# Order of maxima, low parts and prologue changed in an attention and gated-MLP kernel, with GpSimd's low parts in halves

## The chip, the cores and the metric

The kernel runs on one core of one Trainium2 chip. The metric is device time in microseconds (us), lower is better. Before the change three runs gave 1069.33, 1069.58 and 1069.66; their median is 1069.58.

## What is computed

32 heads (4 x 8) of attention over 576 positions with head size 64, in float32, then a gated MLP and a second MLP with a softmax gate and a layer norm:

```python
scores = scale * np.matmul(q, k.transpose(0, 1, 3, 2))
thresh = np.max(scores, axis=-1, keepdims=True) - tau
scores = np.where(scores >= thresh, scores, -1000000000.0)
attn = np.exp(scores - np.max(scores, axis=-1, keepdims=True))
attn = attn / (np.sum(attn, axis=-1, keepdims=True) + 1e-09)
x = np.matmul(attn, v)                      # then laid out as tokens x 512
x = (x @ w_a) * (x @ w_b) @ w_out           # 2304 tokens, 512 -> 1536 -> 512
h = x @ w_in                                # 512 -> 1024
solu = h * softmax(h)
out = layer_norm(solu) * g_ln @ w_out2      # 1024 -> 512
```

The change lies in the attention part only, the first 390 us or so.

## The kernel before

**Numbers in two parts.** Each float32 operand of a product is split into a high part (ScalarE rounds it) and a low part (the rest, by a subtraction). The low part of q and k is made by VectorE (`low_qk`, L811), that of v by GpSimd (`split_v`, L515), that of the probabilities by GpSimd (`low_probs`, L523, 576 columns in one instruction).

**Pairs and slots.** Two heads make a pair, and there are 16 pairs. A head of 576 rows is 4.5 tiles of 128, so a pair is nine slots, 0 to 8: slots 0 to 3 belong to the even head, slots 5 to 8 to the odd one, slot 4 (`MID`) to both and with twice the matmuls. In each slot TensorE does three things in this order (`step` in the tensor block): the scores of a tile one slot ahead (`scores`, for the maxima; in slot 8 that is tile 0 of the pair after the next), the transposed scores of this slot's tile (`scores_t`, for the probabilities), and some matmuls of probabilities and values of earlier tiles (`values`). All this work is 140 matmuls of 288 columns per pair.

**The maxima.** `score_max` (L820) reduces a tile of scores to one column of negated maxima. When a head's tiles are all reduced, ScalarE copies the high parts (`high_max`, L617), GpSimd subtracts to get the low parts (`low_max`, L531), VectorE turns the columns to rows (`turn_max`, L828), and SyncE stores them to DRAM (`store_max`, L352) and loads them back (`load_max`, L357) as two further rows of the operand tile `ops`. So the transposed scores come out with the maximum subtracted.

**Dealing.** `deal` (L341) fills one of four places in `ops` with a head's operands by six DMAs on SyncE's queue: zeros on the two rows of the maxima (`deal_zeros`, L322), the high parts (L328 to L330), the low parts (L338, L339). TensorE waits for all six before it starts the scores of that head: for the even head of pair n+2 in slot 8 of pair n, for the odd head of pair n+1 in slot 3 of pair n. `dealt` counts what has landed.

**The orders.** Each engine has one queue in program order; nothing is reordered. The order is written out by hand in the `step` of each block. SyncE, in a pair e: deal the odd head of e+1, store and load the odd maxima of the pair, load q and k, load v, move a finished head, spread its sums; then deal the even head of e+2, store the even maxima of e+1, load v, load maxima, load q and k, store the inverse, move a head. VectorE turns the odd maxima in slot 0 and the even ones of the next pair in slot 5, ahead of `mask` (L834); `low_qk` stands in slots 2 and 6 (L877, L879), `invert` in slot 7.

**Start and end.** Before the loop TensorE computes the scores of pair 0 alone; the operands of head 0 come straight from the engines, those of the others by `deal`. In slot 8 of pair 14 VectorE also normalizes the first token chunk (`normalize`, L846). Ahead of pair 14 SyncE issues four loads of the inverse sums (`load_inverse`).

Of the kernel before, what the change touches and what calls it, by code (L numbers as in the profile page):

```python
# [16 lines left out]
F32 = mybir.dt.float32  # L17
# [18 lines left out]
def build_program(nc, qkT, v_tiles, tau, w_a, w_b, w_o, w_in, w_out, g_col, eye, out):  # L36
# [35 lines left out]
    with outer:  # L72
# [115 lines left out]
        v_lo_set = sem("v_lo_set")  # L188
        s_done = sem("s_done")
        max_done = sem("max_done")  # L190
        max_hi_done = sem("max_hi_done")
# [104 lines left out]
        def dealt(i, j):  # L296

            return DEALT * (i + j // ROLL + (1 if j % ROLL else 0))

# [6 lines left out]
        def _(sp):  # L306
# [34 lines left out]
            def deal(i, j):  # L341


                at_least(sp, st_done, number(i - 1, j // 2, MID + 1 if j % 2 == 0 else SLOTS))
                deal_zeros(i, j)
                deal_high(i, j)
                deal_low(i, j)
# [50 lines left out]
            def step(i, e):  # L398

                head(deal, i, e + 1, 1)  # L400
                head(store_max, i, e, 1)
                head(load_max, i, e, 1)
                head(load_qk, i, e + 3, 0)
                head(load_v, i, e + 1, 0)

                head(move_head, i, e - 1, 1)
                pair(spread_sums, i, e - 1)

                head(deal, i, e + 2, 0)
                head(store_max, i, e + 1, 0)  # L410
                head(load_v, i, e + 1, 1)
                head(load_max, i, e + 1, 0)
                head(load_qk, i, e + 3, 1)
                pair(store_inverse, i, e - 1)
                head(move_head, i, e, 0)
# [6 lines left out]
            sp.wait_ge(consts_set, CONSTS)  # L422
            deal_zeros(0, 1)
            deal_high(0, 1, qk_hi_done)
            deal_low(0, 1)
            load_qk(0, 2)
            load_v(0, 0)
            deal_zeros(0, 2)
            deal_high(0, 2, qk_hi_done)
            load_qk(0, 3)  # L430
            deal_low(0, 2)
            load_v(0, 1)
            store_max(0, 0)
            load_qk(1, 0)
            load_max(0, 0)
            load_qk(1, 1)
# [57 lines left out]
        def _(pool):  # L494
# [23 lines left out]
            def low_probs(i, e, s):  # L518
                n = number(i, e, s)
                r = (SLOTS * e + s) % RP  # L520
                pool.wait_ge(p_hi_done, n + 1)
                at_least(pool, pv_done, used_up(i, e, s, RP))
                pool.tensor_tensor(p_lo[:, r, :], prob[:, s % RAW, :], p_hi[:, r, :].bitcast(F32),  # L523
                                   ALU.subtract).then_inc(p_lo_done, 1)

# [51 lines left out]
        def _(act):  # L577
# [13 lines left out]
            def exps(i, e, s):  # L591
                n, ps = number(i, e, s), st_ps[(SLOTS * e + s) % 2]
                act.wait_ge(st_done, n + 1)
                at_least(act, p_lo_done, n + 1 - RAW)
                act.activation(halves(prob[:, s % RAW, :]), ps[:, :, 0:HALF], ACT.Exp,  # L595
# [80 lines left out]
            act.wait_ge(consts_set, CONSTS + 3)  # L676
            high_max(0, 0)
            high_qk(0, 3)
# [123 lines left out]
        def _(dve):  # L802
# [58 lines left out]
            def step(i, e):  # L861
                for s in range(SLOTS):
# [3 lines left out]
                    ni, ne = pair_at(i, e + 1)  # L866
                    if s == 0:
                        turn_max(i, 2 * e + 1)
                    if s == 5 and exists(ni, ne):
                        turn_max(ni, 2 * ne)  # L870
                    if s > 0:
                        mask(i, e, s - 1)
                    elif not (isinstance(i, int) and 2 * i + e == 0):
                        mask(*pair_at(i, e - 1), SLOTS - 1)
                    mi, me = pair_at(i, e + 2)
                    if s == 2 and exists(mi, me):
                        low_qk(mi, 2 * me)  # L877
                    if s == 6 and exists(mi, me):
                        low_qk(mi, 2 * me + 1)  # L879
                    if s == 7 and not (isinstance(i, int) and 2 * i + e == 0):  # L880
                        invert(*pair_at(i, e - 1))
# [17 lines left out]
            for s in range(MID):  # L899
                score_max(0, 0, s, first_ps[s % 3])  # L900
            low_qk(0, 2)
            score_max(0, 0, MID, first_ps[MID % 3])
            score_max(0, 0, MID + 1, first_ps[(MID + 1) % 3])
            turn_max(0, 0)
            for s in range(MID + 2, SLOTS):
# [4 lines left out]
            dve.wait_ge(tau_ready, 1)  # L910
            low_qk(0, 3)
            last = heads // ROLL - 1
            for i in range(2):
# [134 lines left out]
        def _(pe):  # L1048
            def product(ps, e, s, weights, moving, done):


                parts = operands(e, s)
                for b in range(2):
# [26 lines left out]
            def values(i, e, side, *parts):  # L1080

                for t, part in parts:
# [5 lines left out]
                    if part == 2:  # L1088
                        pe.wait_ge(p_lo_done, n + 1)
                    elif part == 0:  # L1090
                        pe.wait_ge(p_hi_done, n + 1)
# [51 lines left out]
            for s in range(SLOTS):  # L1143
                at_least(pe, max_done, s - 2)
                scores(0, 0, s, first_ps[s % 3])
            pe.wait_ge(max_done, SLOTS - 2)
            scores(0, 1, 0, first_ps[SLOTS % 3])
# [167 lines left out]
```

## Time and profile before

| | |
|---|---|
| median of three runs | 1069.58 us |
| the profiled execution, its own time | 1069.29 us |
| its span in the trace | 1067.1 us |
| TensorE matmul / weight load busy | 94% / 88% of the span |
| VectorE / ScalarE / GpSimd busy | 51% / 39% / 24% |
| granted TensorE clock, mean | 0.976 |
| DMA packets | 51578, 71.33 MB |

Matmuls are pipelined and their ends are modelled, so the busy share of TensorE is not the share of its peak. 2.2 us of the profiled execution lie outside the span. The attention part ends near 390 us; the stages behind it keep TensorE busy throughout.

### The profile page before, as it was taken

What the parts mean: (1) busy time and instruction counts of PE and PEld (TensorE: products, weight loads), DVE (VectorE), ACT (ScalarE), POOL (GpSimd) and SP (SyncE); (2) the same over time, 40 slices, a digit from 0 to 9 for tenths busy, and PEclk for the clock granted to TensorE, in tenths of its full rate; (3) what the DMA queues carried; (4) which work ended last, traced back from release to release, by engine and by line L of the source; (5) the groups of instructions that cost most, each with busy time, mean ns of one, the idle gap of its engine ahead of it and who ended that gap; (6) DMA issues with size and microseconds to landing.
All of it is one profiled execution on the core that took longest, in us unless ns stands there. A gap on an engine that the chain in (4) does not pass through costs nothing.

```text
span 1067.1 us, 16652 instructions
## 1 busy us (share of the span) xinstructions
PE 1001.3 (94%) x5840; PEld 943.0 (88%) x5840; DVE 543.4 (51%) x862; ACT 415.1 (39%) x739; POOL 252.4 (24%) x242
## 2 busy tenths in 40 slices
PE   4899988999998889999999999999999999999998
PEld 4888878888887879999999999999999978888886
DVE  5676676677677675442122122222223485666564
ACT  2666656566665674431121121211212422322231
POOL 2666666566665670000000000000000000000000
PEclk8999998899999999999999999999999999999999
DMA  5545555454564425421001001000002200000000
GB/s 147 145 119 138 144 124 130 123 139 117 134 148 109 96 75 163 135 60 30 1 1 29 0 0 29 0 0 0 0 0 79 79 10 20 29 20 20 20 30 29
DMA packets 51578, 71.33 MB, mean 67 GB/s; under 512 B 14558, under 2 KB 24926, under 8 KB 51548
## 3 DMA queue, kind: packets, MB, share of 16 engines
q1 hardware_dynamic: 51548, 70.95, 24.9%
q8 instruction: 16, 0.26, 0.1%
q14 instruction: 14, 0.11, 0.0%
HBM read 33.25 MB, written 5.32 MB: 36 GB/s over the span
## 4 chain that ended last, share of the span: by engine, by line
PE 80%; issue 7%; DVE 4%; ACT 3%; DMA 2%; SPq 2%; POOL 2%; DVEq 0%; ACTq 0%; POOLq 0%
PE PS L1111 9%; PE PS L1112 9%; PE PS L1113 9%; PE PS L1094 8%; PE PS L1057 7%; PE PS L1059 5%; PE PS L1177 5%; PE PS L1176 5%; PE PS L1178 5%; PE PS L1235 3%; PE PS L1237 3%; PE PS L1236 3%; PE PS L1211 3%; PE PS L1209 3%; PE PS L1210 3%
## 5 line engine op out<-in xcount | busy, mean ns | idle before, releaser
L523 POOL TENSOR_TENSOR p_lo<-prob,p_hi 128x576 fp32r<-128x576 f32 x144 | 207.3, 1440 | 131.8 <-ACT p_hi L602 131.5
L1057 PE MATMUL PS<-ops 128*128 128x288 f32 x640 | 192.6, 320 | 47.7 <-DVE neg_max L820 29.2
L1111 PE MATMUL PS<-x_hi,w_ab_rolled 128*128 128x384 f32 x576 | 192.5, 334 | 1.4 <-issue 1.4
L1112 PE MATMUL PS<-x_lo,w_ab_rolled 128*128 128x384 f32 x576 | 192.4, 334 | 0.0
L1113 PE MATMUL PS<-x_hi,w_ab_rolled 128*128 128x384 f32 x576 | 192.4, 334 | 0.0
L1059 PE MATMUL PS<-ops 128*128 128x288 f32 x640 | 185.2, 308 | 0.0
L1057 PEld LDWEIGHTS PS<-ops 128*128 128x128 f32 x640 | 129.2, 202 | 61.4 <-DVE neg_max L820 36.4
L931 DVE TENSOR_TENSOR gate<-gate,PS 128x384 f32<-128x384 f32 x72 | 39.9, 554 | 253.0 <-ACT gate L701 253.0
L820 DVE TENSOR_REDUCE neg_max<-PS 128x1 f32<-128x576 f32 x144 | 108.6, 756 | 92.8 <-PE PS L1059 91.6
L701 ACT ACTIVATE gate<-PS 128x384 f32<-128x384 f32 x72 | 35.4, 491 | 268.2 <-PE PS L1113 268.2
L1059 PEld LDWEIGHTS PS<-ops 128*128 128x128 f32 x640 | 129.5, 202 | 0.0
L602 ACT ACTIVATE p_hi<-prob 128x576 fp32r<-128x576 f32 x144 | 98.4, 683 | 72.1 <-DVE prob L834 68.7
L595 ACT ACTIVATE prob<-PS 128x576 f32<-128x576 f32 x144 | 93.2, 647 | 65.3 <-PE PS L1059 63.4
L834 DVE SCALAR_TENSOR_TENSOR prob<-PS,neg_tau,prob 128x576 f32<-128x576 f32 x144 | 115.2, 801 | 2.8 <-ACT prob L595 2.8
L1111 PEld LDWEIGHTS PS<-x_hi,w_ab_rolled 128*128 128x128 f32 x576 | 108.1, 188 | 1.7 <-issue 1.7
L1112 PEld LDWEIGHTS PS<-x_lo,w_ab_rolled 128*128 128x128 f32 x576 | 108.1, 188 | 0.0
L1113 PEld LDWEIGHTS PS<-x_hi,w_ab_rolled 128*128 128x128 f32 x576 | 108.1, 188 | 0.0
L563 POOL MEMSET halfpow<- 128x1 f32 x1 | 0.1, 104 | 448.0 <-PE PS L1178 448.0
L1176 PE MATMUL PS<-g_hi,w_od 128*128 128x384 f32 x288 | 96.2, 334 | 0.0
L1177 PE MATMUL PS<-g_lo,w_od 128*128 128x384 f32 x288 | 96.2, 334 | 0.0
L1178 PE MATMUL PS<-g_hi,w_od 128*128 128x384 f32 x288 | 96.2, 334 | 0.0
L1094 PE MATMUL PS<-p_hi,v_hi 128*65 128x288 f32 x320 | 72.1, 308 | 9.2 <-issue 8.9
(89 smaller groups left out, 1546.8 us busy)
## 6 DMA issues: line engine op xcount, KB each, us to landing
qk_raw<-qkT_dram SPq DMA_DIRECT2D x32, 288.0 KB, 2.8
ops<-qk_hi SPq DMA_DIRECT2D x62, 144.0 KB
ops<-qk_hi SPq DMA_DIRECT2D x31, 288.0 KB
ops<-qk_lo SPq DMA_DIRECT2D x62, 144.0 KB
v_raw<-v_tiles_dram SPq DMA_DIRECT2D x32, 160.0 KB, 2.4
xT<-head_sb SPq DMA_DIRECT2D x32, 144.0 KB, 2.4
out_dram<-o_sb SPq DMA_DIRECT2D x18, 256.0 KB, 2.0
stage<-inverse_dram SPq DMA_DIRECT2D x20, 192.0 KB, 3.8
```

Source lines behind the costliest of these rows:

```text
L523: pool.tensor_tensor(p_lo[:, r, :], prob[:, s % RAW, :], p_hi[:, r, :].bitcast(F32), ALU.subtract).then_inc(p_lo_done, 1)
L820: dve.tensor_reduce(out=neg_max[:, e, s:s + 1], in_=ps[:, :, 0:HALF], axis=AX_XY, op=ALU.max, negate=True).then_inc(max_done, 1)
L834: dve.scalar_tensor_tensor(out=p, in0=ps[:, :, 0:HALF], scalar=neg_tau[:, 0:1], in1=p, op0=ALU.is_ge, op1=ALU.mult).then_inc(mask_done, 1)
L1057: pe.matmul(ps[:, b, 0:HALF], weights[0][:, r, own], moving[0][:, r, cols], start=(n == 0), stop=False)
L1059: ins = pe.matmul(ps[:, b, 0:HALF], weights[1][:, r, own], moving[1][:, r, cols], start=False, stop=(n == len(parts) - 1))
L1094: ins = pe.matmul(o_ps[0:D + 1, b, 0:HALF], v[:, side, t, :], p[:, r, b * HALF:(b + 1) * HALF], start=(t == 0 and part == 0), stop=(t == N ...
L1111: pe.matmul(bank, w[:, 0, :], x_hi[:, k, :], start=(k == 0), stop=False)
L1112: pe.matmul(bank, w[:, 0, :], x_lo[:, k, :], start=False, stop=False)
L1113: ins = pe.matmul(bank, w[:, 1, :], x_hi[:, k, :], start=False, stop=(k == NK - 1))
L1176: pe.matmul(bank, w[:, 0, :], g_hi[:, f % 2, :], start=(f == 0), stop=False)
L1177: pe.matmul(bank, w[:, 0, :], g_lo[:, f % 2, :], start=False, stop=False)
L1178: ins = pe.matmul(bank, w[:, 1, :], g_hi[:, f % 2, :], start=False, stop=(f == NF - 1))
```

## The change

It has five parts.

1. **SyncE's order in the loop.** `store_max` now stands ahead of `deal` in both halves of `step`; `load_max` stands right behind the even `deal`, and `store_inverse` ahead of `load_qk`.
2. **VectorE's order.** `turn_max` of the next pair's even head moves from slot 5 to slot 4, that of its odd head from slot 0 of that pair to slot 8 of this one, both behind `mask`. The second `low_qk` moves from slot 6 to 7, `invert` from 7 to 6.
3. **GpSimd's low parts of probabilities** are made in two instructions of 288 columns, and all who wait for them count to twice the number.
4. **The start.** Heads 1, 2 and 3 get no `deal_zeros`; loads of q and k are issued earlier; four extra matmuls (`product` with `heads_in=1`) and one extra reduce give the last maxima of head 0 without the operands of head 1; `turn_max(0, 0)` and `turn_max(0, 1)` move into the prologue.
5. `dealt` counts five DMAs and not six for heads 1 to 3.

```diff
         def dealt(i, j):
-            return DEALT * (i + j // ROLL + (1 if j % ROLL else 0))
+            return DEALT * (i + j // ROLL) + (DEALT - 16 if j % ROLL else 0)
...
-                deal_zeros(i, j)
+                if not (isinstance(i, int) and i == 0):
+                    deal_zeros(i, j)
...
             def step(i, e):
 
+                head(store_max, i, e, 1)
                 head(deal, i, e + 1, 1)
-                head(store_max, i, e, 1)
                 head(load_max, i, e, 1)
...
+                head(store_max, i, e + 1, 0)
                 head(deal, i, e + 2, 0)
-                head(store_max, i, e + 1, 0)
+                head(load_max, i, e + 1, 0)
                 head(load_v, i, e + 1, 1)
-                head(load_max, i, e + 1, 0)
+                pair(store_inverse, i, e - 1)
                 head(load_qk, i, e + 3, 1)
-                pair(store_inverse, i, e - 1)
                 head(move_head, i, e, 0)
...
-            deal_zeros(0, 1)
+            sp.wait_ge(first_ops, FIRST_OPS)
+            load_qk(0, 2)
             deal_high(0, 1, qk_hi_done)
             deal_low(0, 1)
-            load_qk(0, 2)
+            load_qk(0, 3)
             load_v(0, 0)
-            deal_zeros(0, 2)
             deal_high(0, 2, qk_hi_done)
-            load_qk(0, 3)
+            store_max(0, 0)
             deal_low(0, 2)
+
+            sp.wait_ge(s_done, NT)
+            load_max(0, 0)
             load_v(0, 1)
-            store_max(0, 0)
             load_qk(1, 0)
-            load_max(0, 0)
             load_qk(1, 1)
...
-                pool.tensor_tensor(p_lo[:, r, :], prob[:, s % RAW, :], p_hi[:, r, :].bitcast(F32),
-                                   ALU.subtract).then_inc(p_lo_done, 1)
+                for b in range(2):
+                    cols = slice(b * HALF, (b + 1) * HALF)
+                    pool.tensor_tensor(p_lo[:, r, cols], prob[:, s % RAW, cols], p_hi[:, r, cols].bitcast(F32),
+                                       ALU.subtract).then_inc(p_lo_done, 1)
...
-            high_max(0, 0)
+
+            act.wait_ge(short_max, 1)
+            act.activation(max_cols[:, 0:NT], neg_max[:, 0, 0:NT], ACT.Copy).then_inc(max_hi_done, 1)
...
-                    if s == 0:
-                        turn_max(i, 2 * e + 1)
-                    if s == 5 and exists(ni, ne):
-                        turn_max(ni, 2 * ne)
                     if s > 0:
                         mask(i, e, s - 1)
                     elif not (isinstance(i, int) and 2 * i + e == 0):
                         mask(*pair_at(i, e - 1), SLOTS - 1)
+                    if s == MID and exists(ni, ne):
+                        turn_max(ni, 2 * ne)
+                    if s == SLOTS - 1 and exists(ni, ne):
+                        turn_max(ni, 2 * ne + 1)
...
-                    if s == 6 and exists(mi, me):
+                    if s == 7 and exists(mi, me):
                         low_qk(mi, 2 * me + 1)
-                    if s == 7 and not (isinstance(i, int) and 2 * i + e == 0):
+                    if s == 6 and not (isinstance(i, int) and 2 * i + e == 0):
                         invert(*pair_at(i, e - 1))
...
+            dve.wait_ge(short_done, 1)
+            dve.tensor_reduce(out=neg_max[:, 0, MID:NT], in_=first_ps[2][:, :, 0:HALF], axis=AX_XY, op=ALU.max,
+                              negate=True).then_inc(short_max, 1)
             low_qk(0, 2)
+            turn_max(0, 0)
...
                 scores(0, 0, s, first_ps[s % 3])
+                if s == MID - 1:
+                    pe.wait_ge(max_done, 3)
+                    product(first_ps[2], 0, MID, (qq, qx), (kk, kx), short_done, 1)
```

## Rows read from the trace of the kernel before

**Rows 1.** The page's slices: busy tenths of TensorE in 40 equal parts of the span.

```profile
PE   4899988999998889999999999999999999999998
```

**Rows 2.** Timeline, TensorE: start, us, engine, line, operation, idle before with its releaser.

```profile
44.48 0.40 PE L1057 MATMUL PS<-ops 128*128 128x288 f32 x1 [1.77 <-DVE neg_max L820]
...
217.23 0.29 PE L1057 MATMUL PS<-ops 128*128 128x288 f32 x1
...
229.88 0.40 PE L1057 MATMUL PS<-ops 128*128 128x288 f32 x1 [1.91 <-DVE neg_max L820]
...
232.07 0.71 PE L1094 MATMUL PS<-p_hi,v_hi 128*65 128x288 f32 x2 [0.68 <-issue]
...
345.73 0.40 PE L1057 MATMUL PS<-ops 128*128 128x288 f32 x1 [1.93 <-DVE neg_max L820]
```

**Rows 3.** Windows: stretch, length, busy us by engine, clock, DMA share, GB/s.

```profile
44.48:345.73 301.25, 268.87 (x1821) 254.68 (x1821) 212.07 (x299) 191.42 (x338) 190.66 (x169) 0.94 0.53 131
232.00:232.50 0.50, 0.43 (x2) 0.45 (x3) 0.19 (x1) 0.50 (x2) 0.50 (x1) 0.50 0.00 0
```

**Rows 4.** Timeline of one pair: ScalarE, GpSimd and VectorE around its second low part.

```profile
226.67 0.67 ACT L582 ACTIVATE qk_hi<-qk_raw 128x576 fp32r<-128x576 f32 x1
...
227.12 1.41 POOL L523 TENSOR_TENSOR p_lo<-prob,p_hi 128x576 fp32r<-128x576 f32 x1
...
227.37 1.78 DVE L811 TENSOR_TENSOR qk_lo<-qk_raw,qk_hi 128x576 fp32r<-128x576 f32 x1 [1.33 <-ACT qk_hi L582]
```

**Rows 5.** Timeline, SyncE's queue (SPq: a DMA being issued) in the same pair.

```profile
221.37 0.67 SPq L322 DMA_DIRECT2D ops<-zeros  x1
...
225.67 0.65 SPq L352 DMA_DIRECT2D max_dram<-max_turn  x1
...
232.75 0.67 SPq L322 DMA_DIRECT2D ops<-zeros  x1
```

**Rows 6.** Chain that ended last: two deals whose landing released TensorE (start, us, what).

```profile
142.51 4.10 DMA ops<-qk_lo
...
303.30 0.67 SPq L322
...
306.50 3.38 DMA ops<-qk_lo
```

**Rows 7.** Timeline, GpSimd in the same pair as rows 4.

```profile
220.92 1.43 POOL L523 TENSOR_TENSOR p_lo<-prob,p_hi 128x576 fp32r<-128x576 f32 x1 [1.16 <-ACT p_hi L602]
222.31 0.20 POOL L531 TENSOR_TENSOR max_cols<-neg_max,max_cols 128x5 fp32r<-128x5 f32 x1
```

**Rows 8.** The page's groups: count, busy us, mean ns, idle before; VectorE's reduce and mask.

```profile
L820 DVE TENSOR_REDUCE neg_max<-PS 128x1 f32<-128x576 f32 x144 | 108.6, 756 | 92.8 <-PE PS L1059 91.6
...
L834 DVE SCALAR_TENSOR_TENSOR prob<-PS,neg_tau,prob 128x576 f32<-128x576 f32 x144 | 115.2, 801 | 2.8 <-ACT prob L595 2.8
```

**Rows 9.** Timeline of the start: TensorE and SyncE's queue.

```profile
6.71 0.58 PE L1057 MATMUL PS<-ops 128*128 128x288 f32 x1 [6.71 <-DVE ops L896]
...
10.40 0.59 SPq L310 DMA_DIRECT2D qk_raw<-qkT_dram  x1
...
22.22 0.37 PE L1057 MATMUL PS<-ops 128*128 128x288 f32 x1 [3.12 <-DMA ops<-qk_lo]
...
31.84 0.37 PE L1057 MATMUL PS<-ops 128*128 128x288 f32 x1 [1.46 <-DMA ops<-qk_lo]
```

**Rows 10.** Timeline around pair 14: SyncE's queue, VectorE, GpSimd, TensorE.

```profile
351.86 0.67 SPq L322 DMA_DIRECT2D ops<-zeros  x1
...
370.81 4.40 DVE L846 TENSOR_TENSOR xT<-xT,inverse_first 128x384 f32<-128x384 f32 x4
...
372.60 0.52 POOL L531 TENSOR_TENSOR max_cols<-neg_max,max_cols 128x5 fp32r<-128x5 f32 x1
...
376.08 0.40 PE L1057 MATMUL PS<-ops 128*128 128x288 f32 x1 [1.97 <-DVE prob L834]
```

**Rows 11.** The page's DMA issues: what, count, size, median us to landing.

```profile
v_raw<-v_tiles_dram SPq DMA_DIRECT2D x32, 160.0 KB, 2.4
```

More of the change, by code:

```diff
@@ L189, in build_program @@
         s_done = sem("s_done")
+        short_done = sem("short_done")
+        short_max = sem("short_max")
         max_done = sem("max_done")
@@ L593, in exps @@
                 act.wait_ge(st_done, n + 1)
-                at_least(act, p_lo_done, n + 1 - RAW)
+                at_least(act, p_lo_done, 2 * (n + 1 - RAW))
                 act.activation(halves(prob[:, s % RAW, :]), ps[:, :, 0:HALF], ACT.Exp,
@@ L900, in _ @@
                 score_max(0, 0, s, first_ps[s % 3])
+            dve.wait_ge(short_done, 1)
+            dve.tensor_reduce(out=neg_max[:, 0, MID:NT], in_=first_ps[2][:, :, 0:HALF], axis=AX_XY, op=ALU.max,
+                              negate=True).then_inc(short_max, 1)
             low_qk(0, 2)
+            turn_max(0, 0)
             score_max(0, 0, MID, first_ps[MID % 3])
             score_max(0, 0, MID + 1, first_ps[(MID + 1) % 3])
-            turn_max(0, 0)
             for s in range(MID + 2, SLOTS):
@@ L911, in _ @@
             low_qk(0, 3)
+            turn_max(0, 1)
             last = heads // ROLL - 1
@@ L1048, in _, with product @@
         def _(pe):
-            def product(ps, e, s, weights, moving, done):
-                parts = operands(e, s)
+            def product(ps, e, s, weights, moving, done, heads_in=PAIR):
+                parts = operands(e, s)[:heads_in]
                 for b in range(2):
@@ L1088, in values @@
                     if part == 2:
-                        pe.wait_ge(p_lo_done, n + 1)
+                        pe.wait_ge(p_lo_done, 2 * (n + 1))
                     elif part == 0:
@@ L1144, in _ @@
                 at_least(pe, max_done, s - 2)
+                if s == MID + 1:
+                    pe.wait_ge(short_max, 1)
                 scores(0, 0, s, first_ps[s % 3])
+                if s == MID - 1:
+                    pe.wait_ge(max_done, 3)
+                    product(first_ps[2], 0, MID, (qq, qx), (kk, kx), short_done, 1)
             pe.wait_ge(max_done, SLOTS - 2)
```

## The prediction

> **What bounds the kernel now.** I read the page's slices first [rows 1]. From the sixteenth slice on TensorE is busy throughout; before that it has gaps, and only there does the change touch anything. So the question is the length of a pair. The timeline of TensorE gives it: slot 8 starts at 44.48 in pair 0 and at 345.73 in pair 13 [rows 2], 13 steps of 23.17 us. Over that stretch TensorE is busy 268.87 of 301.25 us and the clock is 0.94 [rows 3].
>
> I then asked of one pair what ends each gap. Call the start of slot 3 S3 (217.23) and the start of slot 8 S8 (229.88) [rows 2]. Up to S8 TensorE stood idle for 1.91 us until VectorE had freed the bank of scores. VectorE was late because its second `low_qk` waited 1.33 us for ScalarE's high part, and then took 1.78 us [rows 4]: GpSimd's low part ran until 227.12 + 1.41 = 228.53, and VectorE ended 0.62 us behind it at 229.15. Behind S8 there is a second gap of 0.68 us [rows 2], TensorE waiting for the copied head, which the same delay made late, and then a stretch at half clock (0.50, the lower level of 1.2 GHz) [rows 3]. All of this is what the reordering of `low_qk` aims at. S3 to S8 is 12.65 us, so S8 to the next S3 is 23.17 - 12.65 = 10.52 on average.
>
> Last I read SyncE's queue, for what would be late next. The even deal starts at 221.37 = S3 + 4.14, the odd one at 232.75 = S8 + 2.87 [rows 5]. In the chain that ended last a deal twice ends a gap of TensorE: first issue at 303.30, last transfer landed at 306.50 + 3.38 = 309.88, 3.20 of issuing and 3.38 of landing, 6.58 us together; in the other the last transfer took 4.10 to land, which makes 7.3 us with the same issuing [rows 6]. So a deal takes 6.6 us at its best, and the odd deal is already nearly on the path.
>
> **Part by part. `low_qk` to slot 7, `invert` to slot 6.** In slot 7 the high part is long there (226.67 + 0.67 = 227.34) [rows 4], so the wait of 1.33 goes, and the reduce that frees the bank stands ahead of it. Without what follows S8 would come 1.9 us sooner, and the copy of the head would no longer be late: -0.6 us on average behind S8. The reduce and a mask stand ahead of `low_qk` in slot 7, so it starts near 228.1 and even at 1.78 us ends at 229.9, before the new S8 of 230.2 (below): it has cover.
>
> **The even maxima ahead of the even deal.** This is what takes it back. `store_max` waits for `turn_max`, which waits for `low_max`, which on GpSimd stands behind the low part of slot 2. `low_max` ends at 222.31 + 0.20 = 222.51 = S3 + 5.28 [rows 7]. I add 0.05 for the split low part, 0.20 for the turn (an estimate, as small an instruction as `low_max`) and 0.05 for hand-overs: the store is issued at S3 + 5.6. It takes 0.65 [rows 5] plus 0.05, and only then come the six DMAs of the deal: first issue S3 + 6.3 where it was S3 + 4.14. With 6.65 us for a deal (6.58 mostly, now and then 7.3) it lands at S3 + 12.97. TensorE needs it in slot 8. So S3 to S8 becomes 12.97 against 12.65: the gap ahead of S8 stays, it only has another releaser. Bounds: 12.9 with 6.58, 13.6 with 7.3.
>
> **The odd maxima ahead of the odd deal.** `turn_max` now stands in slot 8 behind a reduce and a mask. The reduce can start some 0.7 us after S8 (four matmuls); reduce and mask take 0.76 and 0.80 [rows 8], 0.07 less each where the next follows, the turn 0.20, so the store goes out at S8 + 2.35, the deal at S8 + 3.05, about as before (2.87), and lands at S8 + 9.7. TensorE without the late head needs 10.52 - 0.6 = 9.9 us for the same way, half clock included. The larger holds: 9.9. Bounds: 9.7 if the half clock is sometimes missing, 10.4 with the slow deal.
>
> **The pair** is then 12.97 + 9.9 = 22.87 us, 0.30 less than 23.17, times 13 steps: **-3.9 us**.
>
> **Two halves of 288 on GpSimd.** A tile takes 1.43 and the smallest instruction, five columns, 0.20 [rows 7]. A second instruction can add between nothing (all of the time goes by columns) and the whole 0.20. I take 0.05, nearer to the first, since 0.20 holds its own columns and a hand-over; only the pair of halves ahead of `low_max` counts, and it is inside the sum above. VectorE's low parts get shorter by up to 0.7, but they now lie beside a TensorE that waits for a deal: nothing.
> The row shows that VectorE waited for the whole GpSimd instruction. The Trainium skill (SBUF — State Buffer, "SBUF: two separate sides") states the same as an exclusive lock held for a whole instruction; by that rule alone the split would be worth up to 0.7 us of the 1.9 us gap per pair, about 9 us in 13 steps, if `low_qk` were still what the gap waits for, and by the rows above it is worth nothing.
>
> **Turns ahead of later work on VectorE.** The turn in slot 4 waits until S3 + 5.35, and behind it stands the reduce that could start at S3 + 5.2: 0.4 us later, its bank is needed at S3 + 6.6. Covered.
>
> **The start.** The load of head 2 was issued at 10.40; now it goes out when the first operands are ready, just before TensorE's first matmul at 6.71 [rows 9]. Head 0's last maxima come from four matmuls and a reduce at 12 to 13 us, and its store can go near 14. The low part of head 2 goes out some 3 us sooner; TensorE, which waited for it until 22.22 [rows 9], goes on near 19. The next wait, for the deal of head 3, ended at 31.84 [rows 9]; that chain starts 3 us sooner and has one DMA less: -3.2, of which pair 0 gives 0.3 back in its own slots 3 to 8: **-2.9 us** (bounds -2.0 and -3.5).
>
> **The end.** Before pair 14 the odd deal stood behind four loads and started at 351.86 = S8 + 6.13 [rows 10]. Those loads follow `move_head`, which is no longer late; now the deal starts near S8 + 4.9: **-1.2**. But in slot 8 of pair 14 the turn stands ahead of `normalize`. `normalize` began at 370.81 and took 4.40 beside GpSimd [rows 10]; now VectorE waits for `low_max`, which began at 372.60 and with an idle VectorE would end near 372.6. `normalize` starts at 372.8, 2.0 later, and meets less of GpSimd (-0.5). The mask behind it released TensorE at 376.08 after 1.97 us of idle time [rows 10], so this is all on the path: **+1.5**.
>
> **Sum.** -3.9 - 2.9 - 1.2 + 1.5 = -6.5, from 1069.29 of the profiled execution: 1062.8. The median of the runs is 0.3 above it: 1063.
>
> **Rivals.** *Deals land faster* (chance 0.08). The last transfer of a deal, 144 KB, lands 3.4 us after its issue; a load of 160 KB takes 2.4 [rows 11]. If the deal had the engines so much to itself that its last transfer took 2.4, S3 to S8 would be 12.0 and the odd way stays at TensorE's 9.9: 1.0 less per pair, 13 us, 1050. Against it: what fills the DMA engines is the deal itself, and the two landings I can see are 3.38 and 4.10.
> [...]
>
> *An exact exchange* (0.20). If half clock already hid the 0.68 us of the late head, S8 to S3 stays 10.5, a pair becomes 23.5, +4 in the loop, less 2.6 at the ends: 1071. For it: at half clock the two losses lie in the same 3 us.
>
> *Slower, by the deals* (0.12). If all deals take 7.3, the pair is 13.6 + 10.4 = 24.0, +0.8 times 13 = +10.7, less 2: 1078. It decides at 7.0 us per deal: above it the pair is longer than the start gives back. For it: both deals now start later and nearer to the loads behind them; against it: 6.58 behind a `move_head` that was issued right ahead.
>
> *Slower, by the clock* (0.05). A gap of 2.3 us ahead of S8 where 1.9 was, and a second one at S3, could halve the clock for longer: +1 to +1.6 per pair, near 1083.
>
> *The split or the reorder does nothing because VectorE is late anyway* is inside the forecast: with `low_qk` at 1.78 in slot 7 it still ends before S8.
>
> **Chances and range.** The forecast has 0.55. A difference of over 0.2% (2.1 us) is what a measurement of this kernel can tell from none. Faster: the forecast, but for its upper edge, and the first rival, 0.61; same: most of the exchange and that edge, 0.20; slower 0.19. Range: 1055 (between forecast and the fast deals) to 1075 (beyond the exchange, most of the way to the slow deals).
>
> **What would show it.** TensorE's gap ahead of slot 8 released by "DMA ops<-qk_lo" and not by "DVE neg_max L820", still about 2 us long; the first issue of the even deal at S3 + 6.3, right behind a store; the 0.68 us behind S8 gone; S3 to S8 near 13.0, S8 to S3 near 9.9; stretches at half clock about as many as before; GpSimd's halves near 0.74; the first wait of the loop ended near 28.6; `normalize` near 2 us later against slot 8 of pair 14. I am wrong if the gap ahead of S8 is gone (then the maxima turn sooner than GpSimd's row allows, or deals need under 5 us), or if S3 to S8 is over 13.5.

## The result and the profile after

The changed kernel takes 1075.1 us, the median of seven runs (1072.19 to 1077.07); beside it the kernel before takes 1069.66 (seven runs, 1068.54 to 1070.21). The ratio is 1.0048, with a 95% interval of 1.0035 to 1.0061: **slower by 0.5%**. Forecast was 1063, faster, in a range up to 1075.0, so the sign was wrong and the time stands at the very edge, 0.1 us beyond it.

| | before | after |
|---|---|---|
| profiled execution / its span | 1069.29 / 1067.1 us | 1075.1 / 1073.3 us |
| mean granted clock | 0.976 | 0.981 |
| start of slot 8 in pair 0 / in pair 13 | 44.48 / 345.73 | 44.22 / 353.63 |
| one pair between them | 23.17 us | 23.80 us (forecast 22.87) |

In the page the slices answer to [rows 1]: the first sixteen still have gaps, and the rest is untouched. The chain that ended last has changed its make-up: transfers and SyncE's issuing carry 9% each, where they had 2% each. The groups name what TensorE's gaps wait for.

```profile
PE   5789887888889879999999999999999999999998
...
PE 66%; DMA 9%; SPq 9%; issue 7%; DVE 4%; POOL 3%; ACT 2%; POOLq 0%; DVEq 0%; ACTq 0%
...
L530 POOL TENSOR_TENSOR p_lo<-prob,p_hi 128x288 fp32r<-128x288 f32 x288 | 236.3, 843 | 113.9 <-ACT p_hi L609 100.4
L1072 PE MATMUL PS<-ops 128*128 128x288 f32 x642 | 192.4, 319 | 66.2 <-DMA ops<-qk_lo 52.1
```

The timeline of TensorE, first matmuls of slots 3 and 8 (columns as in [rows 2]): the first two are of pair 0, then slot 3, slot 8 and the next slot 3 of the pair used ahead, then slot 8 of pair 13, slot 3 and slot 8 of pair 14, and last the matmul that waits for the mask behind `normalize` (before: 376.08).

```profile
30.26 0.58 PE L1072 MATMUL PS<-ops 128*128 128x288 f32 x1 [3.31 <-DMA ops<-qk_lo]
44.22 0.37 PE L1072 MATMUL PS<-ops 128*128 128x288 f32 x1 [1.96 <-DMA ops<-qk_lo]
...
221.99 0.40 PE L1072 MATMUL PS<-ops 128*128 128x288 f32 x1 [0.83 <-DMA ops<-qk_lo]
235.51 0.40 PE L1072 MATMUL PS<-ops 128*128 128x288 f32 x1 [2.48 <-DMA ops<-qk_lo]
245.55 0.40 PE L1072 MATMUL PS<-ops 128*128 128x288 f32 x1 [1.58 <-DMA ops<-qk_lo]
...
353.63 0.37 PE L1072 MATMUL PS<-ops 128*128 128x288 f32 x1 [2.34 <-DMA ops<-qk_lo]
364.71 0.37 PE L1072 MATMUL PS<-ops 128*128 128x288 f32 x1 [1.12 <-DMA ops<-qk_lo]
375.85 0.40 PE L1072 MATMUL PS<-ops 128*128 128x288 f32 x1 [0.25 <-DVE prob L843]
382.43 0.40 PE L1072 MATMUL PS<-ops 128*128 128x288 f32 x1 [2.62 <-DVE prob L843]
```

The gap ahead of slot 8, 1.91 us behind the reduce in [rows 2], is now 2.48 us behind the deal, and there is a second one ahead of slot 3, also behind a deal. The 0.68 us of the late head are gone. The windows of the same stretch as [rows 3]:

```profile
44.22:353.63 309.41, 264.94 (x1820) 252.91 (x1821) 203.76 (x299) 194.14 (x338) 213.58 (x287) 0.95 0.52 127
```

The 13 pairs take 309.41 us, 8.2 more than 301.25. TensorE's idle part grew from 32.4 (301.25 less 268.87) to 44.5 us, +12.1, and its busy part shrank by 3.9: the same 1820 matmuls, with fewer of them at half clock.

**Where the 6.2 us of span come from:** -0.3 up to slot 8 of pair 0; +8.2 in 13 pairs (+0.63 each); -2.2 from there to slot 8 of pair 14 (22.22 us where 24.42 were); +0.65 for `normalize` in slot 8 of pair 14 (375.85 to 382.43, against 370.15 to 376.08). The four add up to 6.35; what lies behind them is 0.15 shorter.

The chain that ended last runs through every step of one pair; this is its part from the low maxima to the next odd deal (start, us, what):

```profile
227.38 0.17 POOL max_cols L538
...
227.66 0.22 DVE max_turn L837
...
228.04 0.66 SPq L356
...
228.86 0.66 SPq L325
...
232.08 3.39 DMA ops<-qk_lo
...
235.51 0.40 PE PS L1072
...
237.02 0.81 DVE prob L843
...
238.12 0.66 SPq L356
...
238.90 0.65 SPq L325
...
242.11 3.39 DMA ops<-qk_lo
...
245.55 0.40 PE PS L1072
```

GpSimd's last low maxima, the turn (L837), the store (L356), the zeros (L325) as first of six DMAs, the last one landing, TensorE's slot 8; then the mask (L843), turn, store, deal again, and slot 3. TensorE waits for a deal 26 times in the 13 pairs, once ahead of each slot 8 and once ahead of each slot 3, so nothing of this loop has slack: each pair is as long as this chain.

### The profile page after: what moved, and what is told of

It reads as the page before. It is cut to its first block, busy times and chain, and to the rows that moved or that the text cites. A ratio compares the mean times of both kernels' runs of the same rounds, so it can differ in the third digit from the quotient of the medians.

```text
span 1073.3 us, 16908 instructions
## 1 busy us (share of the span) xinstructions
PE 996.3 (93%) x5844; PEld 940.8 (88%) x5844; DVE 532.6 (50%) x863; ACT 418.2 (39%) x739; POOL 279.9 (26%) x386
## 4 chain that ended last, share of the span: by engine, by line
PE 66%; DMA 9%; SPq 9%; issue 7%; DVE 4%; POOL 3%; ACT 2%; POOLq 0%; DVEq 0%; ACTq 0%
PE PS L1126 9%; PE PS L1127 9%; PE PS L1128 9%; DMA ops<-qk_lo 9%; PE PS L1197 5%; PE PS L1198 5%; PE PS L1196 5%; PE PS L1255 3%; PE PS L1072 3%; PE PS L1257 3%; PE PS L1256 3%; POOL p_lo L530 3%; PE PS L1231 3%; PE PS L1229 3%; PE PS L1230 3%
## 5 line engine op out<-in xcount | busy, mean ns | idle before, releaser
L530 POOL TENSOR_TENSOR p_lo<-prob,p_hi 128x288 fp32r<-128x288 f32 x288 | 236.3, 843 | 113.9 <-ACT p_hi L609 100.4
L946 DVE TENSOR_TENSOR gate<-gate,PS 128x384 f32<-128x384 f32 x72 | 39.9, 554 | 253.5 <-ACT gate L710 253.5
L843 DVE SCALAR_TENSOR_TENSOR prob<-PS,neg_tau,prob 128x576 f32<-128x576 f32 x144 | 116.2, 808 | 3.1 <-ACT prob L602 3.0
```

The costliest lines, as they stand in the source:

```text
L530: pool.tensor_tensor(p_lo[:, r, cols], prob[:, s % RAW, cols], p_hi[:, r, cols].bitcast(F32), ALU.subtract).then_inc(p_lo_done, 1)
L843: dve.scalar_tensor_tensor(out=p, in0=ps[:, :, 0:HALF], scalar=neg_tau[:, 0:1], in1=p, op0=ALU.is_ge, op1=ALU.mult).then_inc(mask_done, 1)
```

## The experiments

Each stands beside runs of the kernel before on the same chip. "Waits" is the sum of TensorE's waits from 44 to 345 us; "half clock" is 2 x (1 - mean granted clock) x span, since the clock has only its two levels. Both are of the one profiled execution: other executions of the kernel before have clocks of 0.973 to 0.982, which makes 38 to 58 us of half clock.

| run | median us | ratio (95%) | waits | half clock |
|---|---|---|---|---|
| before | 1069.7 | 1 | 31.7 | 51 |
| after | 1075.1 | 1.0048 (1.0035 to 1.0061) | 43.9 | 41 |
| after, whole tile on GpSimd | 1072.95 | 1.0029 (1.0015 to 1.0042) | 44.2 | 34 |
| after, zeros of even deals last | 1066.86 | 0.9962 (0.9949 to 0.9976) | 39.9 | 30 |
| after, even deal first | 1059.98 | 0.9907 (0.9888 to 0.9926) | 30.6 | 27 |
| after, odd deal first | 1059.52 | 0.9907 (0.9886 to 0.9929) | 34.1 | 38 |
| after, both deals first | 1042.62 | 0.9738 (0.9718 to 0.9757) | 24.8 | 15 |
| the same, whole tile | 1043.06 | 0.9744 (0.9716 to 0.9771) | 24.5 | 15 |
| the same, `low_qk` in slot 6 | 1052.45 | 0.9826 (0.9812 to 0.984) | 29.1 | 23 |
| before + stores first | 1128.35 | 1.0553 (1.0534 to 1.0572) | 60.6 | 103 |
| before + halves on GpSimd | 1058.4 | 0.9876 (0.9841 to 0.9912) | 32.7 | 17 |
| before + `low_qk` in slot 7 | 1036.36 | 0.9689 (0.9669 to 0.9709) | 20.5 | 4 |
| after, deals first, zeros last, later move | 1028.62 | 0.9616 (0.9602 to 0.9631) | 18.3 | 10 |
| the same, earlier copy | 1028.15 | 0.9603 (0.9573 to 0.9632) | 12.4 | 19 |

Three parts of the change were not run alone: the moved turns, the start, and the new places of `load_max` and `store_inverse`.

### Which of the two stores costs: both deals ahead of them

```diff
-                head(store_max, i, e, 1)
                 head(deal, i, e + 1, 1)
+                head(store_max, i, e, 1)
...
-                head(store_max, i, e + 1, 0)
                 head(deal, i, e + 2, 0)
+                head(store_max, i, e + 1, 0)
```

> The changed kernel with each deal put back ahead of its store_max in SyncE's order, all else as changed. Theory A (the deals wait behind the store, the store behind the turn): the even deal starts near S3 + 4.1 again and lands near S3 + 10.8, just when slot 8 can start, and the odd one near S8 + 2.7, landing at S8 + 9.3; a pair takes 20.1 to 20.6 us where the changed kernel has 23.8; 1030 us (1022 to 1040). The gap ahead of slot 8 falls from 2.5 to under 0.5 us. Theory B (the gap is set by VectorE or by the landing itself, and the order of the two on SyncE is of no matter): within 5 us of the changed kernel's 1075.

1042.62 us, 32 less than the changed kernel and 2.6 above the range of theory A. SyncE's queue in one pair:

```profile
228.05 0.68 SPq L325 DMA_DIRECT2D ops<-zeros  x1
...
232.28 0.65 SPq L356 DMA_DIRECT2D max_dram<-max_turn  x1
...
236.80 0.53 SPq L368 DMA_DIRECT2D xT<-head_sb  x1
237.87 0.66 SPq L325 DMA_DIRECT2D ops<-zeros  x1
```

Slot 3 starts at 223.73, the even deal 4.32 behind it and not 6.87, and slot 8 at 234.78, 11.05 behind slot 3. So the wait for the store was the cause. The expectation was 12 us too low; the part that the rows show is that the odd deal does not start at slot 8 itself: it still stands behind `move_head` (L368) and starts at 237.87, 3.09 behind slot 8, little sooner than in the changed kernel (3.39); in this pair TensorE waits 0.66 us for it at 244.76.

One half at a time, the swap of the even pair of lines alone:

> The changed kernel with only the even deal back ahead of its store_max. Theory A: S3 to S8 falls from 13.4 to about 10.8, S8 to S3 stays deal-bound and grows to about 11, since the turn of the odd maxima now waits for GpSimd; a pair 21.8 us, 1049 us (1042 to 1058). Theory B: 1070 to 1080.

and of the odd pair alone:

> The changed kernel with only the odd deal back ahead of its store_max. Theory A: S3 to S8 stays 13.4, S8 to S3 falls from 10.4 to what TensorE needs, 8.9 to 9.9 with the clock; a pair 22.4 to 23.3 us, 1062 us (1057 to 1069). The gap ahead of slot 3 goes, that ahead of slot 8 stays at 2.5 us. Theory B: 1070 to 1080.

The odd one held: 1059.52. TensorE waits only ahead of slot 8 (2.50 and 2.63 us in two neighbouring pairs), the gap ahead of slot 3 is gone. The even one missed, 2 us above its range: with the even deal early, the odd chain is what each pair waits for, at 234.05 with 2.01 us, and the copy of the head is late again in between.

```profile
224.72 0.45 PE L1109 MATMUL PS<-p_hi,v_hi 128*65 128x288 f32 x2 [0.58 <-issue]
234.05 0.40 PE L1072 MATMUL PS<-ops 128*128 128x288 f32 x1 [2.01 <-DMA ops<-qk_lo]
```

So each of the two swapped places costs some 15 us (1075.1 less 1059.98, and less 1059.52), and together they are nearly the 32.

The run with the odd deal first also shows what TensorE needs from slot 8 to slot 3 when no deal holds it, since it waits for nothing there. Two such ways (columns as in [rows 3]) hold the same 63 matmuls without a gap, one at full clock and one that is partly at half clock:

```profile
178.22:186.49 8.27, 8.27 (x63) 8.27 (x63) 5.94 (x9) 5.49 (x9) 5.43 (x9) 1.00 0.69 164
199.94:209.75 9.81, 9.80 (x63) 9.73 (x63) 5.94 (x9) 5.48 (x9) 5.41 (x9) 0.83 0.61 138
```

The way is 8.3 us or 9.8 us long, 9.1 on average over 13 pairs. At a clock of 0.83 some 3.3 us of the 9.81 are half clock, and they cost 1.54, about half of their length.

### What the moved stores cost without the moved low part

The same swap in the other direction, in the kernel before and nothing else.

```diff
-                head(deal, i, e + 1, 1)
                 head(store_max, i, e, 1)
+                head(deal, i, e + 1, 1)
...
-                head(deal, i, e + 2, 0)
                 head(store_max, i, e + 1, 0)
+                head(deal, i, e + 2, 0)
```

> The kernel before with that one part of the change alone: both store_max ahead of their deal on SyncE; VectorE still turns the even maxima in slot 5 and the odd ones in slot 0. Theory A: the even deal starts near S3 + 6.9 and lands at S3 + 13.6 (12.65 before), the odd one waits for the turn in the next pair's slot 0, starts near S8 + 6.5 and lands at S8 + 13.2 (10.5 before); a pair 26.8 us, 48 us slower than before, 1118 us (1100 to 1130). Theory B (the order on SyncE is of no matter): within 5 us of 1070.

1128.35, inside the range: +57.7 us. Here the turns still stand in slots 5 and 0, later than in the change. TensorE's waits from 44 to 345 us (in total, times, longest):

```profile
PE PS L1057 <- DMA ops<-qk_lo: 60.6, 22, 3.5
```

So the store order costs on the kernel before too, nearly twice the 32 us that it costs in the change. That the change's own turns in slots 4 and 8 make the difference is my reading of the two chains; no run moves the turns alone.

### The moved low part alone

```diff
-                    if s == 6 and exists(mi, me):
+                    if s == 7 and exists(mi, me):
                         low_qk(mi, 2 * me + 1)
-                    if s == 7 and not (isinstance(i, int) and 2 * i + e == 0):
+                    if s == 6 and not (isinstance(i, int) and 2 * i + e == 0):
                         invert(*pair_at(i, e - 1))
```

> The kernel before with that one part of the change alone: VectorE's second low_qk in slot 7 and invert in slot 6; GpSimd in whole tiles, SyncE's order and the turns as before. Theory: this takes away the 1.9 us ahead of slot 8 and the late head; then the deals hold both ends as in deal_first (even deal at S3 + 4.1 to + 10.9, odd one near S8 + 2.9, landing at S8 + 9.6), a pair 20.7 to 21.2: 1044 us (1038 to 1052). Rival (the turns in their old slots, or the even maxima behind it, then make TensorE wait): 1056 or more.

1036.36, 1.6 better than the range: two conditions in the kernel before give 33 us. The pair shown takes 21.09 us (219.05 to 240.14); from pair 2 to pair 13 a pair takes 20.74 on average. No gap ahead of slot 8 by `neg_max` is left; the waits are now mostly those for the odd deal and the head.

```profile
219.05 0.40 PE L1057 MATMUL PS<-ops 128*128 128x288 f32 x1 [0.61 <-DMA ops<-qk_lo]
231.68 0.45 PE L1094 MATMUL PS<-p_hi,v_hi 128*65 128x288 f32 x2 [0.31 <-issue]
240.14 0.40 PE L1057 MATMUL PS<-ops 128*128 128x288 f32 x1 [1.15 <-DMA ops<-qk_lo]
```

It is 6 us faster than the changed kernel with both deals first (1042.62). The pairs shown are equally long (223.73 to 244.76 is 21.03), but the average from pair 2 to pair 13 is 21.18 there. In the two profiled executions (spans 1041.8 and 1034.0) slot 3 of pair 0 starts 3.1 us sooner with the changed start (29.67 against 32.73); the next two pairs lose 4.4, the eleven behind them 4.9, pair 13 0.9, and the way from slot 3 of pair 14 to the end of the wait for `normalize` 0.7. So what the changed start gains is lost again by pair 2, and the other parts of the change, taken together, are no gain in the loop.

The counter-test takes the move back in the kernel with both deals first:

> The kernel deal_first with low_qk back in slot 6 and invert back in slot 7. If VectorE's wait for the high part is what held slot 8 in the kernel before, it comes back: S3 to S8 from 11.05 to 12.1 to 12.6 (GpSimd's halves may let VectorE in sooner than the whole tile did), the late head behind S8 too; a pair 22.4 to 23.0, 1058 to 1068 us. If the deals alone set both ends, it stays within 4 us of deal_first, 1043.

1052.45: 10 us are lost, where 15 to 25 were expected. The gap is back, but only 0.88 us long, not 1.9:

```profile
240.17 0.77 DVE L820 TENSOR_TENSOR qk_lo<-qk_raw,qk_hi 128x576 fp32r<-128x576 f32 x1 [1.33 <-ACT qk_hi L589]
...
240.28 2.07 POOL L530 TENSOR_TENSOR p_lo<-prob,p_hi 128x288 fp32r<-128x288 f32 x2
...
241.66 0.40 PE L1072 MATMUL PS<-ops 128*128 128x288 f32 x1 [0.88 <-DVE neg_max L829]
```

`low_qk` waits for the high part for 1.33 us as in [rows 4], but then takes 0.77 and not 1.78. It did not wait for GpSimd's tile, since it began 0.11 us ahead of the first half; it was GpSimd's two halves that took longer, 2.07 together where 1.57 is usual. In other pairs of this run `low_qk` began 0.01 to 0.28 behind the first half and took 1.15 to 1.42. So the 0.77 comes from the order of the two starts and is no measure of the halves.

### What the halves are worth

On the changed kernel, GpSimd back to one instruction of 576 columns:

```diff
-                for b in range(2):
-                    cols = slice(b * HALF, (b + 1) * HALF)
-                    pool.tensor_tensor(p_lo[:, r, cols], prob[:, s % RAW, cols], p_hi[:, r, cols].bitcast(F32),
-                                       ALU.subtract).then_inc(p_lo_done, 1)
+                pool.tensor_tensor(p_lo[:, r, :], prob[:, s % RAW, :], p_hi[:, r, :].bitcast(F32),
+                                   ALU.subtract).then_inc(p_lo_done, 1)
```

> The changed kernel with GpSimd's low part in one instruction of 576 columns again. Theory A: the two halves took 1.53 us up to low_max where one took 1.39, and this lies on the way to the even deal, so S3 to S8 gets 0.14 shorter, nothing else: 2 us faster than the changed kernel, 1073 us. Rival: the halves spare VectorE's low part up to 0.7 us per use on a way that counts, so without them it is over 4 us slower than the changed kernel, 1080 or more.

and the same on the kernel with both deals first:

> The kernel deal_first with GpSimd's low part in one instruction of 576 columns again; low_qk is in slot 7. Theory: low_qk in slot 7 has over 1 us of cover and the way of the even maxima is not that of the even deal here, so the split is of no matter: within 3 us of deal_first's 1042.6. Rival (the split is what makes deal_first fast): 1050 or more.

Both held: 1072.95 (the halves cost some 2 us where they stand in the chain ahead of the store) and 1043.06 (nothing where they don't). The 2 us are as small as the noise, the two intervals in the table overlap; but S3 to S8 in the middle pairs is 13.37 us with the whole tile and 13.51 with the halves, the 0.14 that was expected. On the kernel before, the halves alone:

> The kernel before with that one part of the change alone: GpSimd's low parts in two instructions of 288 columns, and the counts of those who wait. In the kernel deal_first_low6 low_qk in slot 6 took 0.77 between two GpSimd instructions, where it took 1.78 before behind a whole one. Theory: VectorE gets in between the halves, so S8 comes 1.0 sooner per pair and some half clock goes too, until the odd deal, which starts only when the head is moved, holds it: a pair 22.0 to 22.4 where it was 23.17: 1057 us (1053 to 1064). Rival (the halves only add their own time, and the gap ahead of slot 8 is not VectorE's low part): 1068 to 1074.

1058.4, held: -11.6 us. VectorE and GpSimd at the place of [rows 4]:

```profile
223.95 1.33 DVE L813 TENSOR_TENSOR qk_lo<-qk_raw,qk_hi 128x576 fp32r<-128x576 f32 x1 [1.33 <-ACT qk_hi L584]
...
223.87 2.06 POOL L525 TENSOR_TENSOR p_lo<-prob,p_hi 128x288 fp32r<-128x288 f32 x2
...
226.00 0.40 PE L1059 MATMUL PS<-ops 128*128 128x288 f32 x1 [1.45 <-DVE neg_max L822]
```

`low_qk` takes 1.33 where it took 1.78, and the gap is 1.45 where it was 1.91. So the halves have a worth of their own, only not where the first of `low_qk`'s waits has been taken away. The sum of TensorE's waits hardly moved in this run (31.7 to 32.7): 0.46 us less ahead of slot 8, and other waits, for the odd deal and the head, in its place. What fell is the half clock, 51 to 17 us, in all four executions well below the kernel before (clocks of 0.987 to 0.992). That this makes the rest of the 11.6 us is argued, not shown.

### Shortening the deal's own chain

The zeros of even deals issued last, behind the low parts:

```diff
-                if not (isinstance(i, int) and i == 0):
+                if not (isinstance(i, int) and i == 0) and not (j % 2 == 0):
                     deal_zeros(i, j)
...
                 deal_low(i, j)
+                if not (isinstance(i, int) and i == 0) and (j % 2 == 0):
+                    deal_zeros(i, j)
```

> The changed kernel with the zeros of the even deals issued as the last of the six DMAs and not as the first, which takes one issue of 0.7 us out of the way of the data. Theory A: each even deal lands 0.6 to 0.7 sooner, S3 to S8 13.4 becomes 12.8, 14 times: 9 us faster than the changed kernel, 1066 us (1063 to 1069). Rival (the bulk of the landing is a fixed time, the zeros as the last one land just as late): same as the changed kernel, 1075.

1066.86, held: 8 us less than the changed kernel. The chain that ended last shows why: the last to land is the small transfer, 2.62 us behind its issue, where 144 KB took 3.39.

```profile
227.93 0.82 SPq L342
...
228.80 2.62 DMA ops<-zeros
...
231.47 0.40 PE PS L1074
```

With both deals first, the zeros last in every deal, and `move_head` behind the next step's odd deal:

```diff
                 head(deal, i, e + 1, 1)
+                head(move_head, i, e - 1, 0)
...
-                head(move_head, i, e, 0)
...
             step(last, 1)
+            move_head(last, ROLL - 2)
```

> The kernel deal_first, with the zeros last in all deals and the move of the pair's first head behind the odd deal. In deal_first the even deal landed 0.4 late and the odd one at S8 + 10.0 where TensorE needs 8.9. Theory A: both deals land 0.7 sooner, the odd one starts 1 us sooner too; S3 to S8 10.7, S8 to S3 8.9 to 9.0, a pair 19.7 where deal_first has 21.2: 1022 us (1015 to 1032). Rival (TensorE then waits for the maxima, which are loaded later than the deal, or for the head): 1035 to 1043.

1028.62 (1027.79 to 1031.3), inside the range, and 4% faster than both kernels. A pair takes 20.2 us (71.08 to 212.13, seven pairs), not the 19.7 expected. The two moves went in together, so the run does not say what each is worth. In the two pairs around 225 to 245 us TensorE waits for no deal at all; the copied head is what is left.

```profile
224.76 0.45 PE L1110 MATMUL PS<-p_hi,v_hi 128*65 128x288 f32 x2 [0.66 <-issue]
...
244.96 0.45 PE L1110 MATMUL PS<-p_hi,v_hi 128*65 128x288 f32 x2 [0.66 <-issue]
```

To take that wait too, ScalarE copies the head ahead of its next high part:

```diff
+                    if s == SLOTS - 2:
+                        copy_head(i, 2 * e)
...
-                    if s == SLOTS - 1:
-                        copy_head(i, 2 * e)
-                        if exists(ni, ne):
-                            high_max(ni, 2 * ne + 1)
+                    if s == SLOTS - 1 and exists(ni, ne):
+                        high_max(ni, 2 * ne + 1)
```

> The kernel best with ScalarE's copy of the pair's first head ahead of the high part of the probabilities that it stood behind. In best TensorE waits 0.66 us behind slot 8 of each pair for this copy. Theory: the copy ends 0.5 us sooner and nothing else is late next: 15 times 0.5 us, 1021 us (1018 to 1026). Rival (ScalarE's later high part makes mask, low part or the odd maxima late): 1028 or more.

1028.15, no gain: the rival held. The wait for the head is gone, and in its place GpSimd's low maxima come late (`low_max` at 226.82), the turn with them (227.16, VectorE idle for 1.11 us), and so the reduce that frees the bank:

```profile
227.16 0.21 DVE L838 STREAM_TRANSPOSE max_turn<-max_cols 128x32 f32<-128x32 f32 x1 [1.11 <-POOL max_cols L539]
...
228.51 0.40 PE L1073 MATMUL PS<-ops 128*128 128x288 f32 x1 [0.57 <-DVE neg_max L830]
```

## Why the prediction was wrong

**Right: what goes.** `low_qk` in slot 7 finds its high part and takes 0.79 us at 233.14 (0.76 is usual where GpSimd is idle); the reduce no longer waits for it, and neither the gap by `neg_max` nor the late head is left. That the deal takes its place, with "DMA ops<-qk_lo" as releaser, was also right, and so was its length: 228.86 to 235.51 is 6.65 us, as taken from [rows 6].

**Wrong: the start of the even deal.** "The store is issued at S3 + 5.6 ... first issue S3 + 6.3." Measured 6.05 and 6.87 (S3 = 221.99).

```profile
225.80 1.57 POOL L530 TENSOR_TENSOR p_lo<-prob,p_hi 128x288 fp32r<-128x288 f32 x2 [2.05 <-ACT p_hi L609]
227.33 0.20 POOL L538 TENSOR_TENSOR max_cols<-neg_max,max_cols 128x5 fp32r<-128x5 f32 x1
...
227.66 0.21 DVE L837 STREAM_TRANSPOSE max_turn<-max_cols 128x32 f32<-128x32 f32 x1 [1.17 <-POOL max_cols L538]
```

The low maxima end at 227.53, S3 + 5.54 (5.33 taken); of the 0.21, 0.09 are the halves, 1.53 us up to the next instruction where the whole tile took 1.39 [rows 7]. From there to the turn 0.13, from the turn's end to the store 0.17, where I had 0.05 for all hand-overs; from the store to the zeros 0.82 and not 0.70. Six small steps stand in a row, and each hand-over was taken too short. Over the 13 pairs the first issue lies at S3 + 6.29 to + 6.87, 6.67 on average, and the deal takes 6.73 to slot 8, where I had 6.65. S3 to S8 is 13.52 in this pair, 13.40 on average against 12.97: **+0.43**. (The 12.97 was itself a little off: its terms, 5.28 + 0.30 + 0.70 + 6.65, make 12.93.)

**Wrong: the odd deal, and who rules behind slot 8.** Store and deal at S8 + 2.35 and + 3.05, landed at + 9.7, so that TensorE's own 9.9 would rule. In the pair shown 2.61, 3.39 and 10.04 were measured. And where TensorE runs at half clock right behind S8, as in the next pair, the chain is longer, since four matmuls, the reduce and the mask stand in it: slot 8 at 259.06, store at 262.18 (+3.12), zeros at 263.01 (+3.95), slot 3 at 269.73 (+10.67). The window of the way to the store shows it:

```profile
259.06:262.20 3.14, 3.14 (x13) 3.08 (x14) 1.60 (x3) 0.76 (x2) 0.61 (x2) 0.50 0.57 141
```

The first 3 us behind slot 8 are at a clock of 0.50 to 0.55 in nine of the 13 pairs, with the store at S8 + 2.82 to + 3.13, and at 1.00 in four, with the store at S8 + 2.43 to + 2.61. On average the first issue is at S8 + 3.62 and slot 3 at + 10.40, against 9.9: **+0.5**. And the 9.9 was not TensorE's own way: the run with the odd deal first puts that at 9.1. So one term was 0.8 too long and the other 0.7 too short, and in every pair it is the deal that rules. I had used the half clock as part of TensorE's way and forgotten it in the chain of the deal, though the chain begins with TensorE. The two misses together are the 0.93 us between 22.87 and 23.80, 12 us in 13 pairs: the whole difference between 1063 and 1075. That they make it so exactly is luck, since the miss at the start (+2.6) and those at the end (-1.0 and -0.85) below nearly cancel.

**Half right: the start.** Up to S3 of pair 0 it gives 1.6 (31.84 to 30.26), where -3.2 was taken, and pair 0 gives 1.3 of it back (13.96 us from S3 to S8): -0.3 against -2.9. Head 2 is dealt 2.8 us sooner (the last issue at 15.56 and not 18.39), but head 3 only 1.7 (26.56 and not 28.27): its high parts now stand behind the second store, which waits for a turn at 22.83. The same mistake in small.

**Nearly right: the end.** From S8 of pair 13 the deal starts at +3.96 (forecast 4.9), -2.2 against -1.2; `normalize` begins behind its turn and meets less of GpSimd (3.10 us and not 4.40), +0.65 against +1.5.

```profile
378.34 0.21 DVE L837 STREAM_TRANSPOSE max_turn<-max_cols 128x32 f32<-128x32 f32 x1 [1.82 <-POOL max_cols L538]
378.54 3.10 DVE L855 TENSOR_TENSOR xT<-xT,inverse_first 128x384 f32<-128x384 f32 x4
```

**The split.** That it is worth nothing here was right, to within the 2 us that it costs. The halves take 0.81 us each, not the 0.74 of my list. The reason given, that VectorE waits for a whole instruction, is right too, and the run on the kernel before puts a number on it: 1.78 to 1.33 us for each second `low_qk`. There VectorE's low part ends some 0.6 us behind GpSimd's first half, which is 0.81 long, as it ended 0.62 behind the whole tile in [rows 4]. The Trainium skill (SBUF — State Buffer, "SBUF: two separate sides") says that the pair of ports goes to whichever starts first, for the whole of its instruction. The length 1.33 and GpSimd's 2.06 agree, if VectorE takes its turn between the two halves.
I had put up to 9 us on the split where `low_qk` is what the gap waits for, with 0.7 us per pair. That place measured 11.6, but the gap itself gave only 0.46 us per pair, 6 us in 13; that the totals are so near is in part luck.

**The rivals.** Faster deals and slower deals (7.3) are out, with 6.65. The exact exchange came nearest with 1071 and a pair of 23.5, but by another reason: the 0.68 us of the head were not hidden by the half clock, they went, and the odd deal's chain filled their place. Longer half clock is out: 51 to 41 us, less. What the list lacked is the slower side of the forecast's own mechanism: hand-overs up to 0.3 us longer in each half. By my own sum the start and the end give back 2.6 us, 0.2 per pair, so the change turns slower at a pair of 23.37 us, only 0.5 above my 22.87. An error of 0.25 us in each of two chains of six and more steps was enough for the other sign, and I had put a rival on each transfer but none on the hand-overs.

**The table** also tempts to an addition: the change in waits plus half of the change in half clock. From before to after that is +12.2 and -5.2, 7.0 together, measured 6.2 in the span; for both deals first -6.9 and -18.3, measured -25.3; for `low_qk` alone -11.2 and -23.6, measured -33.1. But it is off by 7 us in three runs (the halves on before, the odd deal first, and the run of 1028.62), perhaps since the waits are summed over one fixed stretch, in which the faster kernels do more pairs. And it does not hold between executions of one kernel: of the kernel before, beside the same runs, one has a clock of 0.974 and a span of 1068.1, another 0.982 and 1067.7, where 17 us of half clock less should give 8.5. That half clock costs about half of its length is shown only where TensorE has no gap (8.27 and 9.81 us above); where a deal holds the pair, part of it presumably lies in a way that has to wait anyway; no run changes the half clock alone.

## What to carry to other kernels

Before a DMA that waits for a late result is put ahead of others on an in-order queue, write down who waits for those others: here two swapped lines cost 32 us, as much as the good part of the change (two conditions, alone 33 us on the kernel before) gives. Size such a chain by the distance between starts of neighbouring instructions in the trace, one hand-over per step, and ask whether an engine at half clock stands in it: hand-overs taken some 0.1 us short, several to a chain, and a stretch of half clock that I left out of it were the miss. Know also how long the waiting engine's own way is once nothing holds it: a run with the suspected wait taken away shows it, an average over the old kernel does not. And test the parts of a bundle one by one: three of these parts on the kernel before gave -33, -12 and +58 us.

## What the runs showed of the hardware

**A gap between two GpSimd instructions lets VectorE in.** VectorE's subtraction of two tiles, 576 columns, takes 0.76 us where GpSimd is idle; started 0.25 us into a whole tile of GpSimd it took 1.78, and ended 0.62 behind GpSimd's tile. Started 0.08 us into the first of two halves it took 1.33 and ended some 0.6 behind that half, and the pair of halves took 2.06 where 1.57 is usual. Started 0.11 us ahead of the halves it took 0.77, and the pair 2.07. The cost moves from the one to the other.

**Small instructions on GpSimd.** 288 columns take 0.81 us, and two such instructions 1.53 from the first start to that of the next instruction, against 1.39 for 576 columns at once; five columns take 0.20.

**Half clock.** The same 63 matmuls without a gap take 8.27 us at a clock of 1.00 and 9.81 at 0.83.

**A series of transfers.** Six of them on SyncE's queue, some 0.65 us apart, are all landed 6.6 us behind the first issue; the last, 144 KB, takes 3.39, and a small one in its place 2.62. The Trainium skill (DMA: Bandwidth & Descriptors, "Anatomy of one DMA — SWDGE (gpsimd) path") has about 2.0 us plus bytes over 436 GB/s for a DMA that GpSimd issues, by which 144 KB would take an estimated 2.3 us. These DMAs are issued by SyncE, and no run here issues one from GpSimd; the rows show 1.1 us more, behind five others on the queue.

**The hand-overs of SyncE's queue.** From the end of a turn to the issue of its store 0.17 us in the pair shown, from the start of one DMA's issue to that of the next 0.55 to 0.70 within a deal, and 0.66 to 0.84 from the store to the zeros.
